# Two of the four remainder tiles of x at each batch end are made by GpSimd instead of VectorE, and the loop over whole batches is written out

## The reference

```python
scores = causal(q @ k.T / 8);  a = softmax(scores);  local = a @ v
q_p = where(q > 0, q, exp(q) - 1) + 1
mem_out = (q_p @ M_prev) / (q_p @ z_prev + 1e-6)
attn = g * mem_out + (1 - g) * local            # g = sigmoid(beta), by head
x = attn as (2304 tokens, 512)
x = (sigmoid(x @ w_gate) * (x @ w_val)) @ w_out  # inner width 1536
h = x @ w_in                                     # inner width 2048
out = (h * clip(h + 3, 0, 6) / 6) @ w_out2
```

## Time and profile before

| what | value |
|---|---|
| device time, median of 3 runs | 1131.67 us (1131.20 to 1132.04) |
| the profiled execution, device time | 1132.29 us |
| span of the profiled execution | 1130.5 us |
| PE busy | 1094.5 us (97%) |
| DVE, ACT, POOL busy | 584.8, 559.6, 500.5 us |
| mean granted clock of PE | 0.992 |

### The profile page before, as it was taken

How to read it: one execution, slowest core, us unless ns; L and a number is a source line. 1 busy time by engine, 2 the same in 40 slices (tenths; PEclk the granted TensorE clock), 3 DMA queues, 4 the chain that set the end, 5 groups by cost and what they waited for, 6 DMA issues and landing times.

```text
span 1130.5 us, 21924 instructions
## 1 busy us (share of the span) xinstructions
PE 1094.5 (97%) x6928; PEld 1016.5 (90%) x6928; DVE 584.8 (52%) x1313; ACT 559.6 (50%) x1259; POOL 500.5 (44%) x517
## 2 busy tenths in 40 slices
PE   4998999999999999999999999999999999999998
PEld 3667999998999999999999999898999999899996
DVE  4888757767767768767633333633223232322321
ACT  4776676676776776776754333223323232232322
POOL 5889657656667657657534445991000000000000
PEclk7999999999999999999999999999999999999999
DMA  7551442442442442443222223440000000000000
GB/s 180 127 131 36 128 107 77 118 112 62 112 113 75 123 115 62 117 116 80 66 66 71 81 82 96 124 126 10 28 0 28 0 28 0 0 28 0 28 0 28
DMA packets 100194, 81.36 MB, mean 72 GB/s; under 512 B 7728, under 2 KB 85552, under 8 KB 100144
## 3 DMA queue, kind: packets, MB, share of 16 engines
q1 hardware_dynamic: 100144, 80.77, 26.7%
HBM read 76.03 MB, written 4.72 MB: 71 GB/s over the span
## 4 chain that ended last, share of the span: by engine, by line
PE 86%; DVE 4%; issue 3%; POOL 2%; ACT 2%; DMA 1%; DVEq 0%; SPq 0%; ACTq 0%; POOLq 0%
PE ps L596 81%; PE ps L637 4%; PE ps L651 1%; POOL prob L523 1%; DMA stage<-w_gate 1%; DVE prob L1212 1%; DMA stage<-w_val 1%; DVE phi L1194 1%; POOL WO L510 0%; DVE x_lo L1227 0%; ACT pt_hi L914 0%; DVE znorm_e L1184 0%; DVE znorm L1182 0%; DVE Y L1351 0%; ACT prob L959 0%
## 5 line engine op out<-in xcount | busy, mean ns | idle before, releaser
L596 PE MATMUL ps<-x_hi,WG 128*128 128x288 f32 x1536 | 324.3, 297 | 4.4 <-DVE pt_lo L1160 3.0
L596 PEld LDWEIGHTS ps<-x_hi,WG 128*128 128x128 f32 x1536 | 251.2, 188 | 7.5 <-DVE pt_lo L1160 3.6
L596 PE MATMUL ps<-x_lo,WG 128*128 128x288 f32 x768 | 226.1, 294 | 0.0
L596 PE MATMUL ps<-c_hi,W 128*128 128x384 f32 x768 | 212.0, 339 | 2.8 <-DVE c_lo L1367 2.6
L510 POOL TENSOR_TENSOR WG<-stage,WG 128x512 fp32r<-128x512 f32 x96 | 129.2, 1362 | 119.4 <-ACT WG L942 119.4
L596 PE MATMUL ps<-W,g_hi 128*128 128x512 f32 x576 | 179.0, 391 | 0.0
L1372 DVE SCALAR_TENSOR_TENSOR g_raw<-g_raw,ps 128x384 f32<-128x384 f32 x96 | 53.2, 554 | 218.4 <-ACT g_raw L1104 218.4
L596 PE MATMUL ps<-h_hi,WO 128*128 128x288 f32 x768 | 164.6, 297 | 0.3 <-DVE Y L1351 0.2
L1104 ACT ACTIVATE g_raw<-ps 128x384 f32<-128x384 f32 x96 | 47.2, 492 | 210.5 <-PE ps L596 210.5
L596 PEld LDWEIGHTS ps<-c_hi,W 128*128 128x128 f32 x768 | 141.0, 189 | 7.6 <-DVE c_lo L1367 3.8
L523 POOL TENSOR_SCALAR prob<-prob,rscale 128x128 f32<-128x128 f32 (+4 forms) x160 | 109.1, 700 | 83.9 <-DVE rscale L1172 83.9
(11 more groups left out here) (104 smaller groups left out, 1851.3 us busy)
## 6 DMA issues: line engine op xcount, KB each, us to landing
stage<-w_out SPq DMA_DIRECT2D x64, 256.0 KB, 2.7
qk_st<-qk_t SPq DMA_DIRECT2D x54, 288.0 KB, 4.2
stage<-w_gate SPq DMA_DIRECT2D x48, 256.0 KB, 3.3
stage<-w_val SPq DMA_DIRECT2D x48, 256.0 KB, 3.0
out<-y_out SPq DMA_DIRECT2D x6, 768.0 KB, 3.5
qn_st<-q_n SPq DMA_DIRECT2D x16, 256.0 KB, 3.1
stage<-w_in SPq DMA_DIRECT2D x16, 256.0 KB, 2.7
v_st<-v_n SPq DMA_DIRECT2D x12, 256.0 KB, 2.7
```

Of the source, the lines that this page charges most:

```text
L596: return pe.matmul(o, l, r, start=start, stop=stop, skip_group_check=True)
```

## The change

POOL gets the remainders of the x tiles 1 and 2 and does them between its weight blocks 3 and 4; DVE keeps tiles 0 and 3. A semaphore of its own, `xc_lo_mid`, counts them, and PE waits for both counts. The outer loop in `walk` becomes a Python loop, so its body stands twice in each engine's program, and numbers that were computed in registers from b become constants in the fourth pair of each batch.

```diff
-            with eng.Fori(0, whole) as b:
+            for b in range(whole):
                 with eng.Fori(0, QPB - 1) as q:
                     pair(b * QPB + q + LAG, b * QPB + q, b, q)
                 r = b * QPB + (QPB - 1)
                 pair(r + LAG, r, b, QPB - 1, cut=b + 1)
...
-        LOW_X = {2: (0,), 3: (1, 2), 4: (3,)}
+        LOW_X = {2: (0,), 4: (3,)}
+        MIDDLE_X = (1, 2)
...
+            def middle_x(b):
+                for k in MIDDLE_X:
+                    pool.wait_ge(xc_hi, DT * b + k + 1)
+                    pool.tensor_tensor(x_lo[:, k, :], x_new[:, k, :], x_hi[:, k, :].bitcast(F32), ALU.subtract).then_inc(xc_lo_mid, 1)
+
-            def low_ws(r, p):
-                for slot in CUT[p]:
+            def low_ws(r, p, cut):
+                for i, slot in enumerate(CUT[p]):
+                    if cut is not None and p == 1 and i == 2:
+                        middle_x(cut)
                     for ahead, k in slot:
                         if not ahead or has_next_quarter(r):
                             low_w(r + ahead, k)
...
                 if t == 0:
-                    pe.wait_ge(xc_lo, DT * (b + 1))
+                    pe.wait_ge(xc_lo, (DT - len(MIDDLE_X)) * (b + 1))
+                    pe.wait_ge(xc_lo_mid, len(MIDDLE_X) * (b + 1))
```

More of the change, by code:

```diff
@@ L201, in attention_and_mlps @@
         w_hi, w_done = sem("w_hi"), sem("w_done")
-        xc_hi, xc_lo = sem("xc_hi"), sem("xc_lo")
+        xc_hi, xc_lo, xc_lo_mid = sem("xc_hi"), sem("xc_lo"), sem("xc_lo_mid")
         f_gate, f_val, f_gout, f_vout = [sem(x) for x in ("f_gate", "f_val", "f_gout", "f_vout")]
@@ L463, in _ @@
                          (ld_v, 2 * DMA * FIRST), (v_hi_done, 2 * FIRST), (v_ready, 2 * FIRST),
-                         (ld_m, DMA * FIRST), (m_hi_done, 2 * FIRST), (m_ready, 2 * FIRST), (xc_hi, DT), (xc_lo, DT)):
+                         (ld_m, DMA * FIRST), (m_hi_done, 2 * FIRST), (m_ready, 2 * FIRST), (xc_hi, DT),
+                         (xc_lo, DT - len(MIDDLE_X)), (xc_lo_mid, len(MIDDLE_X))):
                 pool.sem_inc(s, c)
@@ L563, in step @@
                     phi_by_z(n)
-                low_ws(r, p)
+                low_ws(r, p, cut)
             wait_qk(0)
```

## The result

The changed kernel takes 1130.37 us (1128.09 to 1131.52, 13 runs), the kernel before 1131.69 us (1130.20 to 1134.47, 13 runs). The ratio is 0.9983, 95% interval 0.9975 to 0.9991: 1 to 3 us less. The forecast was 1130.2 us.

A forecast was written before the change was run, and what follows sets the result against it. PE was taken to bound the kernel; 1132.29 - 1.33 (loop) + 0.15 + 0.15 (first two ends) - 0.5 (third end) = 1130.8 us, and with the median 0.62 us lower, 1130.2 us. Range 1127.5 to 1132.3, the forecast case's own 1129.4 to 1131.2.

The forecast's parts named there:

- The written-out loop: First batch end: without the outer branch back PE saves 1.33 us, bounds nothing and 1.54 us.
- both holes: PE's holes of 0.91 and 0.63 us at the first batch end, before the products with v and later.
- Its second part: The loop's register arithmetic that turns into constants was costed at nothing, on queues of engines that wait for PE.
- The moved hole: First two batch ends: POOL holds m_hl, so the hole before G0 moves to O6, growing from 0.28 to 1.84 us.
- G0's delay of 0.15 us: At each of the first two batch ends G0 starts 0.15 us later than in the kernel before.
- The rival with `m_hl` not held: First two ends: both G0 holes close, 2.0 to 2.8 us; in all 3.8 to 4.6 us saved; chance 0.17.
- The third end: No m_hl follows the last attention pair, so PE starts G0 0.5 us sooner, bounds 0 and 0.78.
- Late fetch: DVE's inner-loop branches back fetch late: 1133.3 us with one copy hit, 1136 with two; with other slower courses 0.10.
- The sum: All terms together: 1132.29 - 1.33 + 0.15 + 0.15 - 0.5 = 1130.8 us for the profiled execution.

The follow-up runs named there:

- e1_loop_only: The kernel before with only the outer loop written out, all remainders left on DVE; ratio 0.9996 (0.9987 to 1.0004).
- e5_before_early_c: The kernel before with the second layer's first chunk meant to be split before the first layer's last two sums; 1131.13 us, ratio 0.9990.
- e8_loop_registers: e1_loop_only, but the fourth pair of each batch takes its numbers from a register again (a loop of one turn); 1130.54 us, one execution.
- e3_mhl_last: The changed kernel with both m_hl remainders at the first two batch ends moved to the end of slot 4, where POOL is idle; 1127.34 us, ratio 0.9950.
- e2: The changed kernel with the outer loop put back, so only the two remainders moved to POOL; ratio 0.9993 (0.9985 to 1.0002).
- e9_before_c_earlier: e5_before_early_c with ACT waiting only for the last value unit and DVE's four remainders ahead of sum O0; 1126.99 us, ratio 0.9945.

## Why the prediction was right, point by point

**The written-out loop** was priced at 1.33 us and measured 1.53 at its place (e1_loop_only), near the upper bound of 1.54, which took in both holes. Against the first end of e5_before_early_c (3.30 us) it would be 1.76. Its second part, that constants in place of register arithmetic bring nothing, is open: 0.25 us more came off at the second end, and e8_loop_registers neither confirms nor clears that cause.

**The moved hole** was right in mechanism and size. Predicted: `m_hl` for 2.0 us, a hole of 1.84 us before O6, none before G0. Measured: 1.87 us, 1.62 and 1.60 us, none. G0's delay of 0.15 us at each of these ends was not there: against e1_loop_only the move saves 0.10 us at each. With the move alone it was 0.31 us lost at the first, beside the branch, and 0.12 saved at the second. At the second end one detail differs: POOL had to wait 0.97 us for the high part of block 5, so DVE's x tile 3 took 0.76 us and not 1.5. It changed nothing, for PE was the later one, as worked out. The size of O6's hole, 0.2 us under the forecast, follows the hold, 1.87 us and not 2.0. The rival with `m_hl` not held is refuted by its rows, and e3_mhl_last shows what it would have been worth in the batch section: 2.45 us.

**The third end**: 0.5 us predicted, 0.53 in the changed kernel (the hole of 0.78 us is 0.25). This term was right.

**Late fetch** did not occur: from 100 to 580 us DVE has no gap ascribed to "issue" longer than 0.53 us in the changed kernel, in any of the three inner loops.

**The sum** put the batch section's gain at 1.5 us; it is 2.53 us. By way of e1_loop_only this is 1.81 us for the written-out loop, where 1.33 was forecast, and 0.72 us for the move, where 0.2 was forecast. Nearly the whole miss of 1.0 us is the second end's 0.25 us, the 0.2 us by which the first end's branch was underpriced, and the first two ends, which the move made 0.2 us shorter together and not 0.3 us longer; each was small, and all went one way. The time at the end came out on the forecast because something that it did not have worked the other way: the change of layer, where 1.8 us went back in the profiled executions. So a part of the agreement of 1130.2 with 1130.37 us is luck. The base is another uncertainty: the medians differ by 1.3 us, and the ratio of the runs puts the gain at 1.9 us.

## What to carry to other kernels

Before you move a subtraction from VectorE to GpSimd, list what VectorE does beside its new place. Here the operations there with two SBUF inputs waited for GpSimd's subtractions, even those of 0.2 us: two in a row took 1.87 us. So put the small ones where GpSimd is idle. Measure a small gain in the stretch it was made in, by marks of the bounding engine, and not only by the end of the program: a pause elsewhere with its own fall of the clock can swallow or add more than the gain. At one far branch back VectorE stood without work for 2.13 to 2.82 us in the four kernels that have it (before, e2, e5, e9); writing out the loop of two turns removed it.

## What the runs showed of the hardware that I had not expected

The granted clock fell to half after short pauses too, and not each time. In e9_before_c_earlier it did so after the G0 hole of the first end, which exists in the kernel before without that effect:

```profile
270.65 0.19 PEld L596 LDWEIGHTS ps<-x_hi,WG 128*128 128x128 f32 x1 [1.44 <-DVE pt_lo L1160]
```
```profile
271.00:276.00 5.00, 5.00 (x28) 4.98 (x27) 2.10 (x9) 1.97 (x6) 1.00 (x3) 0.66 0.07 19
```

The clock is 0.66 over these 5 us, after a hole of 1.44 us; the same hole in e1_loop_only (1.44 us) had none after it. The first end of e9_before_c_earlier still cost only 3.25 us: DVE's gap of 2.13 us at the branch stands, but PE, at half clock, is busy for all of these 5.00 us and has no hole for it. And fills of POOL, 1.1 us each, leave DVE's two-input operations alone, while its two subtractions (3.31 us together) hold even a 64x64 one of 0.2 us.
